# Attention and expert kernel: the first load of v in five parts, other transfers held behind it, TensorE's opening work reordered

## What is computed

```python
def _attn_ref(u, v, z):                      # u, v: 8 x 3072 x 256, z: 8 x 3072 x 64
    scores = (1.0 / S) * np.matmul(z, z.transpose(0, 2, 1))
    attn = np.maximum(scores, 0.0) ** 2
    out = np.matmul(attn, v)
    return (u * out)

def _moe_ref(x, w_gate, w1, w2, capacity):   # x: the 24576 rows; the routing runs in order of rows
    logits = x @ w_gate
    ...
    # argmax expert, softmax weight of it, place pos in that expert's queue of `capacity` rows, kept if free
    h = np.maximum(np.einsum('ecd,edf->ecf', disp, w1), 0.0)
    y = np.einsum('ecf,efd->ecd', h, w2)
    # out row i = gate weight * y of its expert and place, zero where it was not kept
```

## Time and profile before

| what | value |
|---|---|
| device time, three runs | 886.87, 886.45, 885.63 us; median 886.45 |
| the profiled execution | 889.07 us |
| its span in the trace | 887.3 us, 22840 instructions |
| mean granted TensorE clock | 0.996 of full |
| busy: TensorE | 867.8 us (98%) |
| busy: VectorE | 630.9 us (71%) |
| busy: ScalarE | 572.1 us (64%) |
| busy: GpSimd | 120.2 us (14%) |
| moved by DMA | 97.87 MB, mean 110 GB/s |

### The profile page before, as it was taken

The page is one execution under the profiler, slowest core; times in us unless marked ns, Lnnn a source line. Parts: engine busy times, 40 slices in busy tenths (PEclk is TensorE's granted clock), DMA queues, the critical chain, the costliest instruction groups (busy, mean ns, idle before and its releaser), DMA issues.

```text
span 887.3 us, 22840 instructions
## 1 busy us (share of the span) xinstructions
PE 867.8 (98%) x7397; PEld 690.7 (78%) x7398; DVE 630.9 (71%) x1346; ACT 572.1 (64%) x871; POOL 120.2 (14%) x119
## 2 busy tenths in 40 slices
PE   5999999999999999999999999999899999999997
PEld 4877787887788888888888888888677777777776
DVE  6976867888888888788888887677255565655531
ACT  6968776768768669787777876777144344434422
POOL 0001102101101101110110110110112112121212
PEclk8999999999999999999999999999999999999999
DMA  9955619624633650110111012411714245225100
GB/s 287 205 190 179 195 36 348 195 57 139 195 89 107 232 178 20 51 41 24 42 53 25 28 51 55 168 42 35 166 42 150 54 130 166 84 94 154 51 20 35
DMA packets 105991, 97.87 MB, mean 110 GB/s; under 512 B 63869, under 2 KB 94666, under 8 KB 104816
## 3 DMA queue, kind: packets, MB, share of 16 engines
q1 hardware_dynamic: 101072, 84.92, 32.9%
q0 software_dynamic: 4896, 12.64, 4.0%
HBM read 40.03 MB, written 44.93 MB: 96 GB/s over the span
## 4 chain that ended last, share of the span: by engine, by line
PE 91%; DMA 3%; issue 2%; ACT 1%; SPq 1%; DVE 1%; POOL 0%; ACTq 0%; POOLq 0%; DVEq 0%
PE O L642 16%; PE O L646 15%; PE O L644 15%; PE Sc L755 14%; PE Sc L607 8%; PE Sc L608 8%; PE O L776 3%; PE O L778 3%; PE O L780 3%; DMA rawv<-in_v 2%; PE M L778 2%; PE M L776 2%; PE M L780 2%; ACT Sc L432 1%; PE M L682 1%
## 5 line engine op out<-in xcount | busy, mean ns | idle before, releaser
L646 PE MATMUL O<-vS,attn_lo 128*128 128x256 f16 x1332 | 363.0, 273 | 0.0
L642 PE MATMUL O<-vS,attn_hi 128*128 128x256 f16 x1332 | 363.0, 273 | 0.0
L644 PE MATMUL O<-vS,attn_hi 128*128 128x256 f16 x1332 | 363.0, 273 | 0.0
L913 DVE TENSOR_TENSOR attn_lo<-attn,attn_hi 128x768 f16<-128x768 f32 x224 | 214.7, 958 | 7.7
L432 ACT ACTIVATE Sc<-Sc 128x768 f32<-128x768 f32 x224 | 178.2, 795 | 51.7 <-PE Sc L608 41.3
L436 ACT ACTIVATE attn<-Sc 128x768 f32<-128x768 f32 x224 | 181.7, 811 | 7.1
L607 PE MATMUL Sc<-zP 128*128 (+1 forms) x450 | 147.3, 328 | 7.0 <-ACT attn L436 5.3
L642 PEld LDWEIGHTS O<-vS,attn_hi 128*128 128x128 f16 x1332 | 130.3, 98 | 27.6 <-DVE ubuf L952 1.0
L644 PEld LDWEIGHTS O<-vS,attn_hi 128*128 128x128 f16 x1332 | 130.3, 98 | 26.5
L907 DVE CAST attn_hi<-attn 128x768 f16<-128x768 f32 x224 | 125.3, 560 | 34.1 <-ACT attn L436 30.3
L608 PE MATMUL Sc<-zQ,zP 128*128 (+1 forms) x450 | 147.0, 327 | 0.0
(11 more groups left out here) (147 smaller groups left out, 891.1 us busy)
## 6 DMA issues: line engine op xcount, KB each, us to landing
out<-empty SPq DMA_DIRECT2D x8, 3072.0 KB, 11.7
wraw<-in_moe_w SPq DMA_DIRECT2D x16, 1024.0 KB, 7.7
rawv<-in_v SPq DMA_DIRECT2D x12, 768.0 KB, 11.6
ubuf<-in_u SPq DMA_DIRECT2D x19, 384.0 KB, 3.2
disp<-empty SPq DMA_DIRECT2D x8, 774.0 KB, 17.8
rawz<-in_z SPq DMA_DIRECT2D x3, 768.0 KB, 6.3
rawv<-in_v SPq DMA_DIRECT2D x1, 1024.0 KB, 7.5
rawv<-in_v SPq DMA_DIRECT2D x1, 896.0 KB, 9.2
```

Of the source, the lines that this page charges most:

```text
L642: nc.tensor.matmul(o_part(t), hi, v[:, 0:D], start=c == 0 and j == 0 and t % 2 == 0, stop=False, skip_group_check=True)
L644: nc.tensor.matmul(o_part(t), hi, v[:, D:2 * D], start=False, stop=False, skip_group_check=True)
L646: ins = nc.tensor.matmul(o_part(t), lo, v[:, 0:D], start=False, stop=c == PAIRS - 1 and j == 1, skip_group_check=True)
L913: dve.tensor_tensor(attn_lo[:, b, :, :], attn[:, b, :, :], attn_hi[:, b, :, :], ALU.subtract).then_inc(s["lo_done"], 1)
```

## The change

The load of v of batch 0 is cut into five parts of 4, 6, 6, 5 and 3 chunks instead of four of 8, 7, 5 and 4; a fifth semaphore and a fifth partial sum go with it. SyncE waits for the fifth part before it issues w_gate, and with it everything behind: u, the fills of `disp`, z and v of batch 1. On TensorE, 56 and 28 constant products stand where 40 and 20 stood. In group 0 the values of pair 0 come before the scores of pair 3 instead of behind them; all other pairs keep their order. Line numbers shift by one to four in the changed kernel.

```diff
--- before.py
+++ after.py
@@ -176,7 +176,7 @@
 
             return (Oa[:, 0, 0:D], Mp[:, 0, 0:D], Oa[:, 1, 0:D])[t]
 
-        names = """consts empty_ready loaded_z00 loaded_z01 loaded_wg loaded_v0a loaded_v0b loaded_v0c loaded_v0d
+        names = """consts empty_ready loaded_z00 loaded_z01 loaded_wg loaded_v0a loaded_v0b loaded_v0c loaded_v0d loaded_v0e
             zsq0 v_high vparts0 vsum0 nrm0 mx0 amx0 scales0 vsum_done nrm_psum nrm_done zhi_ready khi_ready zlo_ready klo_ready loaded_zv loaded_u loaded_w0 loaded_w1
             scores_ready relu_done square_done hi_done lo_done o_ready
             evac_done row_free l1_ready rscale_ready rows_hi rows_lo loaded_xT logits_ready gmx_ready gamx_ready wgs_ready g_step below_ready exp_ready
@@ -238,9 +238,10 @@
             for h in range(2):
                 sp.dma_start(rawz[:, h * SLICE * P:(h + 1) * SLICE * P], z[0, :, h * SLICE * P:(h + 1) * SLICE * P]
                              ).then_inc(s[f"loaded_z0{h}"], 16)
-            for q, name in enumerate("abcd"):
+            for q, name in enumerate("abcde"):
                 sp.dma_start(rawv[:, V0_PIECES[q]:V0_PIECES[q + 1], :], v[0, :, V0_PIECES[q]:V0_PIECES[q + 1], :]
                              ).then_inc(s["loaded_v0" + name], 16)
+            sp.wait_ge(s["loaded_v0e"], 16)
             sp.dma_start(wg[:, :, :], w_gate).then_inc(s["loaded_wg"], 16)
 
             def load_expert(e, par):
@@ -408,8 +409,8 @@
                 return act.activation(dump, rawv[:, bass.ds(at, chunks), :].rearrange("p c d -> p (c d)"),
                                       ACT.Abs, scale=1.0 / SUM_SCALE, accum_out=vsum[:, bass.ds(column, 1)])
 
-            for q in range(SLICES):
-                act.wait_ge(s["loaded_v0" + "abcd"[q]], 16)
+            for q in range(len(V0_PIECES) - 1):
+                act.wait_ge(s["loaded_v0" + "abcde"[q]], 16)
                 v_sum(q, V0_PIECES[q], V0_PIECES[q + 1] - V0_PIECES[q]).then_inc(s["vparts0"], 1)
                 act.wait_ge(s["vparts0"], q + 1)
 
@@ -621,9 +622,9 @@
             wait_keys(2, False)
             scores(0, 0, 0, 0)
             scores(1, 0, 1, 0)
-            turn_over(40)
+            turn_over(56)
             scores(2, 0, 2, 0)
-            turn_over(20)
+            turn_over(28)
 
             end, stop0, stop1, stop, low = (pe.alloc_register(f"pe_{name}") for name in
                                             ("end", "stop0", "stop1", "stop", "low"))
@@ -656,7 +657,8 @@
                             if peeled and (c + LEAD) % PSLICE == 0:
 
                                 wait_keys(2 * ((c + LEAD) // PSLICE) + 2, False)
-                            scores(K0 + c + LEAD, n, c + LEAD, par)
+                            if not peeled or c:
+                                scores(K0 + c + LEAD, n, c + LEAD, par)
                         else:
                             if c + LEAD == PAIRS:
 
@@ -697,6 +699,8 @@
                                     ins = nc.tensor.matmul(M[1][:, 32:32 + E], ones[:, :], onehot[:, k, :],
                                                            start=k == 0, stop=k == TILES - 1)
                                 ins.then_inc(s["counts_ready"], 1)
+                        if peeled and c == 0:
+                            scores(K0 + LEAD, n, LEAD, par)
                         if not peeled and c == NORMS_AT:
                             def next_norms():
                                 wait_apart(pe, s["norm_step"], (n & 120) + 8)
@@ -921,8 +925,8 @@
             first_z(0)
             first_z(1)
             first_z(2)
-            dve.wait_ge(s["vparts0"], SLICES)
-            dve.tensor_reduce(mx[:, 1:2], vsum[:, 0:SLICES], AX.X, ALU.add).then_inc(s["vsum0"], 1)
+            dve.wait_ge(s["vparts0"], len(V0_PIECES) - 1)
+            dve.tensor_reduce(mx[:, 1:2], vsum[:, 0:len(V0_PIECES) - 1], AX.X, ALU.add).then_inc(s["vsum0"], 1)
             dve.wait_ge(s["amx0"], 1)
             link(v_bits())
             link(v_back())
@@ -1235,7 +1239,7 @@
 
 
 HPAIRS = 4
-V0_PIECES = (0, 8, 15, 20, 24)
+V0_PIECES = (0, 4, 10, 16, 21, 24)
 SUM_SCALE = 2.0 ** 13
 SUM_AT = (6, 7, 8, 9)
 W_MAX_AT = (6, 7, 8, 9)
```

## The result

The change makes the kernel slower: 893.59 us (median of six runs, 889.90 to 894.58) against 886.49 beside it (six runs, 885.63 to 888.19), ratio 1.0073 [1.0052, 1.0093], or 7.1 us at the medians. The forecast was 887.6, in a range of 883.0 to 889.8, with 0.28 on slower; the time lies outside.

A forecast was written before the change was run, and what follows sets the result against it. TensorE, 98% busy, was held by batch 0's v load and SyncE's wait for batch 1's load. A 0.3 us gain less 1.5 of clock makes 1.2 slower, from 886.45 to 887.6 us; range 883.0 to 889.8.

The forecast's parts named there:

- the second place: At 66 us, second group: SyncE waits 11.8 us for batch 1's v before xrow's transposes; TensorE's logits wait 0.6 us.
- The sums: ScalarE's sums of |v| in the opening: last one ends at 15.9, so relu(0) comes 2.3 us earlier.
- 56 and 28 constant products: TensorE's opening: clock taken as kept, values ahead of the fourth scores, first values at 20.07, lead 3.6 us.
- rival 1: The lead is kept: batch 1's load little or not later, SyncE free by 57.2; faster, 883.7 at no shift; chance 0.26.
- What is moved later: w_gate, u and eight fills start later, so batch 1's z and v land 2.4 us later, at 59.2.
- the bound of 3.3: Upper limit, in us, of the shift of the fills, if all sixteen DMA engines share one limit.
- rival 2: SyncE's wait for batch 1's later load takes more than the change gives; 889.1 at a 3.3 us shift; chance 0.20.
- Five parts, nothing behind them: Load of batch 0's v: last part lands at 14.4 in place of 17.0, as the fills are held back.
- rival 3: Opening: v's parts land no earlier, last at 17.0, fills from 19.5; slower, 890.8; chance 0.08.
- The added 24 constant products lie in idle time: TensorE's opening: the extra products run in idle time or ahead of the wait for v's low half.
- Everything behind 67 us is the same program with the same waits: After the second group's logits nothing was to differ, so no term was counted there.
- The clock after that wait: TensorE behind its 3.9 us wait for the transposes: half clock costs 0 to 2.05 us, taken as 1.5.

The follow-up runs named there:

- The kernel without the hold: Changed kernel without SyncE's wait for the fifth part before w_gate, u and the fills, the rest of the change kept: 887.11 us, ratio 1.0014.
- without the hold and with 60 products: Changed kernel without SyncE's wait for the fifth part, and 60 for 72 constant products where TensorE leaves the attention loop: 886.02 us, ratio 0.9990.
- the products alone: Unchanged kernel with 56 and 28 constant products for 40 and 20, nothing else: 886.7 us, ratio 1.0000.
- the second trace of after from the first chip: Changed kernel word for word, run once more on the first chip against the unchanged kernel: 889.89 us, ratio 1.0048.
- the hold alone: Unchanged kernel plus SyncE's wait for the fourth part of v before w_gate, u and the fills: 885.95 us, ratio 0.9992.

## Why the prediction was wrong

**What held.** The mechanism of the second place: SyncE comes out of its wait for the load of batch 1 later than VectorE's rows are ready, TensorE stands still with its lead (62 to 66.95), and its clock is at half behind it (not so in the two later traces of after, with waits of 0.6 and 1.8 us). In the opening the fifth part lands at 14.55 (forecast 14.4), relu(0) is at 15.60 (15.9), the third scores at 17.29 at full clock (17.6), the first values at 19.90 (20.07). *The sums*, *56 and 28 constant products* and rival 1's rejection all stand.

**Step "What is moved later": the shift of 2.4 us.** It was 4.3: the load landed at 61.09, not 59.2, beyond the bound of 3.3. "Part of the 3.3 comes back, since nobody starts with a lag now" was wrong; nothing came back, and the fills' issue took 19.9 us. A part of it is the start. w_gate moves from 15.5 on and u from 16.0, as forecast,

```profile
15.50:16.00 0.50, 0.29 (x6) 0.11 (x3) 0.47 (x3) 0.47 (x2) 0.00 (x0) 1.00 0.17 17
```

but the fills' packets (1032 B, so under 2 KB) come from 17.6 on, not from 16.9. From 16.9 to 17.6 us there is none, from 17.6 to 18.1 there are some 100:

```profile
DMA packets 65, 0.20 MB, mean 285 GB/s; under 512 B 0, under 2 KB 0, under 8 KB 65
```

```profile
DMA packets 134, 0.17 MB, mean 342 GB/s; under 512 B 14, under 2 KB 111, under 8 KB 134
```

Before they began at 13.5, so they start 4.1 us later and not 3.3, and the load of batch 1 is 4.3 later. w_gate's first byte comes 0.9 us behind the start of its issue (14.57, 0.33 long) and 0.6 behind its end; I had counted 1.3 from the start. The Trainium skill, page "DMA: Bandwidth & Descriptors", section "Specifications", gives 0.6 us to the first byte, and the trace agrees if it is counted from the end of the issue. In pairs of traces from one chip the last packets of batch 1's load end 3.0 us later with the change (second chip, 53.1 and 56.1) and 3.5 later (first, 54.1 and 57.6), so the 2.4 was too small everywhere. The prediction had one trace of the fills and so no idea that their rate differs by a fifth between executions of one kernel; that is rival 2, and it came out beyond its own price (the transposes 1.6 us later than before, not 0.6).

**Step "Five parts, nothing behind them": the gain of 2.3 us.** The trace had one DMA engine lagging until 17.0. That was an exception. The last sum of two further traces of the unchanged kernel:

```profile
14.72 1.06 ACT L408 ACTIVATE vS<-rawv 128x1024 f16<-128x1024 f32 x1
```

```profile
13.51 1.06 ACT L408 ACTIVATE vS<-rawv 128x1024 f16<-128x1024 f32 x1 [0.41 <-DMA rawv<-in_v]
```

relu(0) follows at 15.90 and 14.69, the first values at 21.67 and 20.42, against 24.35 in the earlier trace rows and 19.90 with the change. The kernel without the hold has 15.10 and 19.66, as early as with it. It is not always so: without the hold and with 60 products the last sum waited until 15.28, relu(0) came at 16.25 and the first values at 21.19. Over all traces the last sum starts between 14.2 and 15.1 with the hold, and between 13.5 and 17.0 without. So the hold brings nothing to a usual opening; whether it spares the late ones is not shown. TensorE's lead over a usual execution of before, less the 0.65 of the moved scores, is thus 0 to 1.1 us, not 3.6. So rival 3, given 0.08, was right in its point (the parts usually land no earlier for it) and wrong in its reason (they are not late either). By its size this covers the 2.6 us by which the profiled execution of before stood over its median, and it is why I think the medians differ by more than the traces. The prediction knew of these 2.6 and moved its sum over unchanged, though an execution that far off has some stall which the usual one hasn't.

**Step "The added 24 constant products lie in idle time" and "Everything behind 67 us is the same program with the same waits".** Both are true of the time in which the products run, and false of the program. They lengthen it by 48 instructions, and a 16 KB block of them is fetched in front of the experts' transposes: 2.3 us more of wait (2.7 us of wait in the kernel with the products alone), and 2.2 to 2.6 us in the time. No rival had this.

**Step "The clock after that wait": 1.5 us.** It was 2.2, just over the long end (2.05).

By these, the loss over a usual execution of before on such a chip: 5.0 of waiting and 2.2 of clock, 2.3 at the experts, less a lead of 0 to 1.1, is 8.4 to 9.5. The trace of after stands 8.4 (span 892.2) over the one of 883.8 on the second chip, and 9.6 over the one of 882.6 on the first; the medians of the result say 7.1.

**What stays open.** The clock's 2.2 us was read from a trace, not isolated by a run. So was its part in the price of the early block. Why one DMA engine lagged in the first trace of before wasn't tried. What sets the rate of the fills is open; it differs between chips and between executions. After itself did not run on the third, where the fills were slow. That the fetch delays the transposes by holding one DMA engine is read from its packet and from the second transpose's issue; the runs show only that its place in the program decides.

## What to carry to other kernels

Where one engine waits in program order for a load that is needed much later, ahead of a transfer that is needed soon, count its slack against the slowest rate of the queue, not against one trace; moving the wait behind the near work cost nothing here (ratios 0.9998 and 1.0005). An execution above its kernel's median is no base for a stall in the opening: the stall may be the very thing that puts it there. And instructions that run in idle time aren't free where their number moves an instruction fetch into a critical transfer.

## What the runs showed that was not expected

- A block of 16 KB of instructions is one DMA packet of 1.1 to 1.7 us at that place. When it falls among the DMA transposes, the next one's issue takes 2.5 to 2.9 us instead of 1.4, and their reader waits 2.3 to 3.0 us instead of 0.3 to 0.5. (In the second trace of after from the first chip it came earlier, 1.3 us behind the first issue, and it was the issue of the copy in between that took 1.16 us instead of 0.57.)
- A longer wait is not a longer time by as much. The early block adds 2.2 us of wait and takes away 1.4 of a later one; the fallen clock decides whether that gain is kept.
- Eight stores of 774 KB each in rows of 1032 bytes take 16.5 to 19.9 us to issue with the hold, by chip and execution, for the same program.
- The clock in the opening of one and the same kernel differs from run to run: in before it was at half from 18 to 21.5 in one trace, behind 2.7 us of idle time, and never in another, whose waits there were 1.5 us at most (below). But a wait of 1.8 us for `xT` was followed by the half clock with the hold alone (64.6 to 68.0) and not in the second trace of after from the first chip.

```profile
18.00:20.00 2.00, 2.00 (x19) 1.77 (x18) 1.97 (x4) 1.97 (x4) 0.00 (x0) 0.52 1.11 249
```

```profile
18.00:20.00 2.00, 0.55 (x8) 0.34 (x6) 1.85 (x3) 1.97 (x4) 0.00 (x0) 1.00 1.12 227
```
